# Attention, mixture of experts and MLP on one core: scores before transposes in each step of TensorE

## What is computed

```python
scores = scale * np.matmul(q, k.transpose(0, 1, 3, 2))
thresh = np.max(scores, axis=-1, keepdims=True) - tau
scores = np.where(scores >= thresh, scores, -1000000000.0)
scores = scores - np.max(scores, axis=-1, keepdims=True)
attn = np.exp(scores)
attn = attn / (np.sum(attn, axis=-1, keepdims=True) + 1e-09)
return np.matmul(attn, v)
```

## Time and profile before

| what | us |
|---|---|
| median of 3 runs | 1074.06 (1073.38 to 1075.02) |
| profiled execution | 1071.44 |
| its span, first to last instruction | 1069.4 |
| busy in the span: TensorE | 985.5 |
| weight loads | 836.9 |
| VectorE | 488.7 |
| ScalarE | 448.6 |
| GpSimd | 228.5 |

### The profile page before, as it was taken

The page is one execution under the profiler, slowest core; times in us unless marked ns, Lnnn a source line. Parts: engine busy times, 40 slices in busy tenths (PEclk is TensorE's granted clock), DMA queues, the critical chain, the costliest instruction groups (busy, mean ns, idle before and its releaser), DMA issues.

```text
span 1069.4 us, 18245 instructions
## 1 busy us (share of the span) xinstructions
PE 985.5 (92%) x5702; PEld 836.9 (78%) x5703; DVE 488.7 (46%) x1071; ACT 448.6 (42%) x1015; POOL 228.5 (21%) x350
## 2 busy tenths in 40 slices
PE   6999999999997289999995957999999999999997
PEld 5777877877874268888884747989999999999996
DVE  6877877877886542121122324642223223222221
ACT  4777877877874032222223224432232222222222
POOL 5655555555541000011000011010000100100000
PEclk8999999999999589999999987999999999999999
DMA  4232222232511271111110523111020110100101
GB/s 89 48 69 55 56 66 54 56 66 54 186 41 24 94 260 48 39 39 49 40 49 29 186 74 84 60 50 30 1 59 0 29 29 0 44 15 1 30 1 29
DMA packets 99968, 59.72 MB, mean 56 GB/s; under 512 B 83680, under 2 KB 83680, under 8 KB 99936
## 3 DMA queue, kind: packets, MB, share of 16 engines
q1 hardware_dynamic: 92800, 43.82, 15.5%
q0 software_dynamic: 3040, 9.96, 3.2%
q10 hardware_dynamic: 4096, 5.54, 1.4%
HBM read 40.95 MB, written 18.35 MB: 55 GB/s over the span
## 4 chain that ended last, share of the span: by engine, by line
PE 83%; DVE 5%; issue 4%; POOL 3%; DMA 2%; ACT 1%; ACTq 1%; DVEq 0%; SPq 0%; POOLq 0%
PE s_ps L1357 19%; PE s_ps L1340 12%; PE s_ps L1274 10%; PE o_ps L1293 10%; PE o_ps L1185 7%; PE o_ps L1340 6%; PE s_ps L1171 6%; PE pt_ps L1137 6%; PE pt_ps L1151 2%; DVE probs L684 1%; PE s_ps L1282 1%; PE pt_ps L1326 1%; PE pt_ps L1264 1%; POOL qk_parts L551 1%; POOL k_swap L561 1%
## 5 line engine op out<-in xcount | busy, mean ns | idle before, releaser
L933 DVE TENSOR_TENSOR g<-s_ps,sig 128x384 f32<-128x384 f32 x96 | 53.5, 557 | 276.8 <-ACT sig L1109 276.8
L1109 ACT ACTIVATE sig<-s_ps 128x384 f32<-128x384 f32 x96 | 47.2, 492 | 284.7 <-PE s_ps L1357 284.7
L724 DVE TENSOR_SCALAR_CACHE_REDUCE scores<-s_ps,taus 128x576 f32<-128x576 f32 x144 | 117.8, 818 | 63.4 <-PE s_ps L1171 41.4
L1357 PE MATMUL s_ps<-yT_high,w_in_high 128*128 (+1 forms) x384 | 132.2, 344 | 1.4 <-DVE yT_low L907 1.2
L684 DVE SCALAR_TENSOR_TENSOR probs<-scores,thresh,probs 128x576 f32<-128x576 f32 x144 | 131.0, 911 | 0.0
L1137 PE MATMUL pt_ps<-ident,probs 128*128 128x128 f32 x720 | 126.7, 277 | 4.1 <-ACT pT L958 2.7
L1357 PE MATMUL s_ps<-yT_high,w_in_low 128*128 (+1 forms) x384 | 130.3, 339 | 0.0
L1357 PE MATMUL s_ps<-yT_low,w_in_high 128*128 (+1 forms) x384 | 129.6, 338 | 0.0
L995 ACT ACTIVATE probs<-scores,row_low 128x576 f32<-128x576 f32 x144 | 115.5, 802 | 10.6 <-DVE scores L724 9.0
L1171 PE MATMUL s_ps<-qkT 128*128 128x288 f32 x320 | 102.6, 337 | 2.6 <-DVE k_swap L678 0.5
L1137 PEld LDWEIGHTS pt_ps<-ident,probs 128*128 128x128 f32 x720 | 84.0, 140 | 26.5 <-issue 19.5
(11 more groups left out here) (181 smaller groups left out, 1877.9 us busy)
## 6 DMA issues: line engine op xcount, KB each, us to landing
w_raw<-in_moe_w_dram SPq DMA_DIRECT2D x16, 512.0 KB, 4.6
y_dram<-slot_y ACTq DMA_DIRECT2D x19, 256.0 KB, 2.0
x_dram<-xs SPq DMA_DIRECT2D x16, 288.0 KB, 2.8
out_dram<-out_sb SPq DMA_DIRECT2D x36, 128.0 KB, 2.4
qk<-in_q_dram SPq DMA_DIRECT2D x32, 128.0 KB, 2.2
w_in_raw<-in_moe_w_in_dram SPq DMA_DIRECT2D x4, 1024.0 KB, 5.0
w_out_raw<-in_moe_w_out_dram SPq DMA_DIRECT2D x16, 256.0 KB, 2.6
qk<-in_k_dram SPq DMA_DIRECT2D x30, 128.0 KB, 2.4
```

The source lines that it names most:

```text
L724: dve.tensor_scalar(scores[:, i % SCORE_SLOTS].rearrange("p (c n) -> p c n", c=2), s_ps[i % 2][:, :, 0:HALF], taus[:, 3:4], None, ALU.mult ...
L1357: mm = pe.matmul(mlp_h_ps[f % 2], w_part[:, a, f * P:(f + 1) * P], y_part[:, bass.ds(c % 2 * DB + a, 1)].rearrange("p a b -> p (a b)"), st ...
```

## The change

In `step` of TensorE, `score` is now called first in every step, not only in the first two; the transposes follow. `values` and `turn` stay at the end of their steps. All semaphores, waits, operands and counts are the same.

```diff
-                    first = isinstance(quad, int) and n < 2
-                    if first:
+                    if on(n, 0, UNITS):
                         score(n, i, quad)
                     if on(n, LAG, UNITS + LAG) or on(n, 0, UNITS - U):
                         transpose(n + U, (i - LAG) % STEPS, 1 - j, u, on(n, LAG, UNITS + LAG), on(n, 0, UNITS - U))
-                    if on(n, 0, UNITS) and not first:
-                        score(n, i, quad)
                     if u in (1, 5) and on(pair, 1, PAIRS + 1):
                         values(last_quad, last_j, 0 if u == 1 else 1)
```

## The result

The changed kernel has a median of 1078.64 us (1076.48 to 1078.98), beside 1074.80 (1072.12 to 1077.14) of the kernel before in the same comparison: ratio 1.0035, 95% interval 1.0019 to 1.0051, so +3.8 us (+2.0 to +5.5). The forecast was +1.95: the sum had the direction right and the size short by half. "Within 0.2%" had been held a little likelier than "slower" (0.49 against 0.43); the ratio is 0.35% up, and its interval starts at 0.19%. One execution of the kernel before (1742 us) and the profiled one of e7_after_swap5 (2367 us) fell in a far slower state and are not used.

The account below looks back on a forecast made before the run. TensorE's issue order in the attention stage was taken as the bound. Fourteen pairs of heads gave +1.7 us, the start −0.4 and the end +0.65: +1.95 on 1074.06, so 1076.0 us, range 1071.0 to 1082.0.

Parts of the forecast that it names:

- Short burst: Steps 2 to 5, between starts of two values blocks: +0.10 us a pair on 9.29, bounds 0 to +0.20.
- joint V to S: Scores starting right behind a values block: taken as 0.03 us, bounded at 0 to 0.10.
- the double score stands between T4 and T5 and covers that one: Today step 4's eight score matmuls cover ScalarE's copy between transposes 4 and 5; afterwards that gap is 1.37 us, +0.05 to +0.07.
- The joint T to V: Values block starting behind step 5's or 1's transposes: costs +0.11 us, against +0.07 behind scores; start to start 0.88.
- faster rival: Joints to values and turn cost nothing and the key swap no longer delays step 0's scores: 1070.4 us, chance 0.10.
- Long burst: Steps 6 to 1, between starts of two values blocks: 10.77 to 10.80 us against 10.78, so +0.02 a pair.
- the wait in front of T0: Step 0's scores wait 0.4 us for the key swap with its transposes queued behind: these start at 5.68, not 5.34.
- The splits keep more slack than now: GpSimd's splits of the next keys: finished with more time to spare than today; no size given.
- Start: First pair, up to the first values block: VectorE's third reduction up to 1.1 us earlier; −0.4 us, bounds −1.1 and +0.7.
- End: Last burst of the attention stage: transposes about 0.55 us later behind scores, plus a joint, so final values +0.65 us.
- joints at their upper bounds: Slower rival, joints between groups at highest cost: +0.35 us a pair, +5.2 in all, 1079.2 us, chance 0.14.
- Wait in front: Slower rival: GpSimd's chain not brought forward, step 0's scores wait: long-burst interval 11.61 us, whole 1087.3, chance 0.10.

Follow-up runs that it names:

- e7_after_swap5: Changed kernel with GpSimd's key swap for the next pair moved from step 6 to step 5, ahead of the split: 1078.41 us, ratio 1.0041.
- e5: Changed kernel with the middle unit's queries and keys copied by one instruction instead of three, part of the attention not computed: 1079.35 us, ratio 1.0051.
- e1_short: Kernel before, with scores first only in steps 2 to 5, from the second pair on: 1079.63 us, ratio 1.0052.
- e2_long: Kernel before, with scores first only in steps 6 to 1, not in the first pair: 1086.07 us, ratio 1.0117.
- e12: Changed kernel with GpSimd's key swap moved to the end of step 5, behind the split: 1077.61 us, ratio 1.0042.
- e6: Kernel before, with GpSimd's key swap moved from step 6 to step 5, ahead of the split: 1075.76 us, ratio 1.0014.
- e3: Kernel before, with scores first only in the first eleven units (first pair and two steps of the second): 1073.83 us, ratio 1.0003.
- e8: The changed kernel once more, unaltered, beside the kernel before: 1077.58 us, ratio 1.0052.
- e10: Kernel before, with GpSimd's key swap moved to the end of step 5, behind the split: 1071.21 us, ratio 0.9984.
- e11: Kernel before, with the key swap behind step 5's split and ScalarE's exponential of step 8 issued behind step 0's copies: 1069.84 us, ratio 0.9971.

## Why the forecast was right in direction and short in size

*Short burst: mis-sized, the failed term.* The forecast came to 9.39, measured is 9.60. By the distances of the trace (V to T2, T2 to T3, T3 to T4, T4 to T5, T5 to V) the forecast's own terms are 3.39, 1.37, 2.35, 1.37 and 0.88, and measured are 3.47, 1.37, 2.37, 1.36 and 1.02. (These terms add up to 9.36; the forecast had added small changes to 9.29 instead and came to 9.39.) Three terms hold to 0.02. S2 to T2 is 0.63 where 0.55 was taken, 0.52 for the scores and 0.03 for the joint V to S; 0.11 above the scores' 0.52 is also just outside the bound of 0.10. It is no joint of V: S0 to T0 and S8 to T8 take 0.63 and 0.64 too, and S0 to T1 took 0.63 before (110.89 to 111.52). The forecast had split a T and its S into 0.78 and 0.52. By the starts, T to S takes 0.68 (108.08 to 108.76) and S to T 0.63, so an S that stands alone behind V costs more than its share of the sum. The larger miss is the last term: 0.14, of which e5 gives back 0.13. The sentence "the double score stands between T4 and T5 and covers that one" was read as covering the first copy only. What T5 waits for is two things: `keys_copied`, for its first four blocks, and `turned_copied`, for its queries and keys; the second is later after the middle unit, which alone has three copies. I priced each gap by a typical step. The step that loses its cover had to be priced by its own instructions.

*The joint T to V: right.* 0.88 was taken, with the earlier trace rows behind it, and the steady part shows 0.89 (114.48 to 115.37). The weight loads don't take it off. Weight-load row of the changed kernel at that joint:

```profile
115.36 0.74 PEld L1185 LDWEIGHTS o_ps<-pT,vv 128*64 128x64 f32 x8 [0.17 <-issue]
```

The first load of V starts with V and not under the transposes before it. The faster rival's joints at no cost were not there. "TensorE: Matmul & The Clock Gate" of the Trainium skill, section on the array's architecture, says that TensorE's queue can pull weight loads ahead of matmuls in flight; at this joint the trace doesn't show it.

*Long burst: right, in part by luck.* Forecast 10.77 to 10.80, measured 10.77 (10.72 to 10.78). VectorE's earlier queue start, GpSimd's chain and the swap came in at 4.97 after V's end, 0.11 earlier than forecast. e1_short and e2_long show the chain by taking away half of it. But two misses cancel: T0 stands 5.60 after V's end (forecast 5.68), and T0 to T1 takes 1.44 (forecast 1.37). T8 came 0.08 later than forecast, by the 0.63 above, and with it ScalarE's round: its copy of T8 starts at 112.12, a round of 1.58 later is 113.70, and the copy of T0 starts at 113.75, with no idle time before it. The forecast had let the wait in front of T0 set T1. T0 itself would have allowed it at 113.68 (113.04 + 0.64). So the wait and the round end almost together, and e12, which takes the wait away, gains 0.03.

*"The splits keep more slack than now": holds, though no row stood behind it.* Step 5's split is through 2.45 before T0's queries and keys start in the kernel before (107.82, 110.27) and 4.2 before in the changed one (109.25, 113.47). Step 2's has 0.32 before and 1.8 after. e6 shows how little the 0.32 is.

*Start: right on the mechanism, missed the clock.* VectorE's third reduction came at 16.96 instead of 17.89, 0.93 earlier ("up to 1.1"); with the scores ahead it is at 16.94 to 17.07 in the four profiles read (changed kernel, e3, e8, e12), with the old order at 17.89 to 18.41 in four others (before, e1, e2, e6). What that is worth at the first V isn't shown: 32.55 and 32.45 with the new order where the clock held, 32.60 to 33.25 in the six with the old one. Not foreseen was that S9 in front of T9 leaves TensorE idle 1.91 in one piece, and that the clock fell behind it in four of six profiles. In the changed kernel's it turned −0.4 into +1.1, 0.4 beyond the bound of +0.7.

*End: right.* +0.65 forecast; from the V 14 pairs after the first to the last V it grew by 0.71, of which 0.57 in the burst that holds the last scores (9.57 to 10.14).

*The scale.* The last V is 6.3 us later by the two profiles, 5.2 of it in the steady part and the end. The medians differ by 3.8 in one comparison (ratio 1.0035) and by 3.7 in another (e8, ratio 1.0052), and the intervals of the two ratios overlap. So the total came out nearer to the forecast than the stage did, and why isn't shown. Behind the last V the profiled executions need 730.7 us (before) and 731.9 (changed); over all experiments it is between 730.7 and 736.3, though nothing there differs. That part scatters more than this change is worth. The distance from the first V to the one 14 pairs later repeats far better (284.85 and 284.73 in the two profiles of the changed kernel, 280.34 and 280.33 in the kernel before and e3_first), and the readings above rest on such distances.

Of the rivals, "joints at their upper bounds" (1079.2) is nearest to the time, and its bound of +0.20 on the short burst was exceeded (+0.31). But the larger part of the miss, 0.14, lay in ScalarE's copies and in no joint. "Wait in front" was the right price for the wrong kernel: e2 pays it, the full change doesn't.

## What to carry to other kernels

When two groups of work on the busiest engine swap places, list for each gap between the users of a shared buffer what covers it before and after, and price the release by the instructions of that very step: an odd step (here three copies instead of one) shows only once its cover is gone. Split the time of two groups by the starts of both, in the order in which they will stand: the same scores took 0.63 here, where 0.55 had been read out of a sum. Where a queue on another engine starts with one of the groups, changing the order in part of the steps can cost far more than changing it in all (1.0117 against 1.0035). And taking a visible wait away pays only as far as the next one: at most 0.03 us a pair in one order (e12), 0.1 in the other (e10), and more came when ScalarE's exponential was moved out of its round as well (e11).

## What the runs showed of the hardware that was not expected

- The granted clock fell behind 1.90 to 2.31 us without a matmul in four executions, to 0.50 in the 3 us of the changed kernel's shown above, and stayed at 1.00 behind 1.89 and 1.65 us in two others with the same order. In the middle of the stage, with a steady mix of transposes, scores and values, it is 1.00.
- Where a VectorE mask met a GpSimd split or key copy for 0.5 us or more (kernel before and changed kernel, 40 to 310 us), the one that started second grew, and the one that started first kept its length. In the changed kernel a mask started at 110.94 keeps its 0.81, and the key copy started at 111.08 lasts 1.20 instead of 0.66. In e6 a key copy started at 199.42 keeps its 0.66, and the mask started at 199.46 lasts 1.23; the split's second half started at 190.19 lasts 1.56, as it does in the changed kernel (107.69) with hardly a mask beside it, and the mask started at 190.52 lasts 1.83. So a step moved on one of the two engines moves durations on the other.
- A group of values behind a group of transposes starts 0.20 after the start of the last transpose (124.76 to 124.96), a group of scores 0.03 behind (123.23 to 123.26 in the same burst). What makes the 0.20 isn't shown by any run here; it recurs at each such joint.
